# A mixing layer and two feed-forward layers on one core: features laid on the rows, with no turning on TensorE

## The chip, the cores and the metric

The kernel runs on one core of a Trainium2 chip. The metric is the device time in microseconds (us) of one execution. The kernel before takes 1403.92 us, the median of three runs (1402.54 to 1404.48). The profiled execution, from which all rows here come, took 1403.23 us, and its span from the first to the last instruction is 1401.4 us.

## The reference, cut to what matters

8192 tokens (2 sequences of 4096) of 192 features, in float32. First a causal mixing over 7 taps: 8 heads of 24 features each share a softmax weight for each tap. Then two feed-forward layers, 192 to 2048 to 192, with different functions between the two products.

```
w   = softmax(weight_gen over k)                  # [tokens, 8 heads, 7 taps]
mix[s, h, g] = sum_k w[s, h, k] * x_pad[s + k, h, g]   # 6 zero rows ahead of each sequence
h   = mix @ w_in1                                 # [8192, 2048]
g   = (a0 + a1 h + a2 h^2 + a3 h^3) / (1 + |b0| |h| + |b1| h^2 + 1e-6)
x2  = g @ w_out1
h   = x2 @ w_in2
y   = (h * clip(h + 3, 0, 6) / 6) @ w_out2
```

## The kernel before

**Precision by splitting.** TensorE is fed float32 values split into a rounded part ("hi") and the rest ("lo"). A product into a hidden layer is five matmuls of 128x128 by 128x512 (`first_product`, L502 to L506): hi by hi, hi by lo, lo by hi, and two for the features beyond 128 ("tail"). A product out of a hidden layer is five more (`second_product`, L510 to L514), into the two banks `acc_a` and `acc_b`. The tail rows carry the 64 features beyond 128 twice, so that one matmul does the work of two.

**Tiles and stages.** The tokens are cut into 16 blocks of 512. A block's hidden layer of 2048 is cut into 16 chunks of 128. Time is cut into segments `s` of 16 steps `c`. In segment `s` layer 1 works on block `s + 1` and layer 2 on block `s`, six chunks behind (`SHIFT`). Each full step so issues 20 matmuls: 5 into and 5 out of layer 1, 5 into and 5 out of layer 2. In segment -1 there is only layer 1 of block 0, and beside it the weights of layer 2 are loaded and split, and the mixing weights of all later tokens are normalised. Segments 1 to 12 are a hardware loop of two segments a turn, so 6 turns and 5 jumps back, on every engine; the others are unrolled.

**What a step does on the engines.** ScalarE (ACT): `den_num_start` reads the hidden chunk out of PSUM twice (L671, L672), `den_absolute` (L677), `den_log` (L682) and `recip_estimate` (L688) make a reciprocal as exp(-ln Q), `g1_round` (L695) and `g2_round` (L703) round the hidden activations, `gate_start` (L710) is layer 2's relu. VectorE (DVE): `den_sign` L843, `horner_v` L851, `horner_w` L858, `recip_t` L866, `recip_m` L874, `quotient` L885, and layer 2's `gate_h` L894. GpSimd (POOL): the two rests `g_lo`, L446 and L455. Each engine works strictly in the order in which its instructions are written out in `for c in range(NC)`; every hand-over is a semaphore.

**What a block adds.** Tokens are laid out with 4 tokens of each block on each of the 128 partitions, features along the row. POOL mixes in that layout: 7 products (L397) and 6 sums (L406, L411, L412), the weight of a head read again for each of its 24 features. TensorE then turns the mixed tile (`turn_mixed`, L615, 8 transposes), ACT and DVE round and subtract (L746, L916). The layer-1 sums are copied by ACT (L723, L726), the second bank is folded by a matmul with the matrix `fold` (`fold_layer1`, L577), and split (L731, L908). The result of layer 2 is copied (L716, L717), turned back (`turn_result`, L593 and L594, in steps 10 and 11), copied again (L740) and stored. All turned tiles pass through one PSUM bank, `turn`.

**PSUM.** There are eight banks: two each for `acc1` and `acc2`, two for `h1`, one for `h2`, one for `turn`. A layer-1 chunk occupies its `h1` bank from its first matmul until `quotient` has read it: TensorE's `layer1_in` waits for the quotient of two chunks before.

**Queues.** All DMAs are issued by SyncE (SP) on one queue in program order: per block one load of `x_win` and one store.

Of the kernel before, what the change touches and what calls it, by code (L numbers as in the profile page):

```python
# [7 lines left out]
F32 = mybir.dt.float32  # L26
# [4 lines left out]
TPB = 4  # L31
BLOCK = P * TPB
SHIFT = 6
Q_ONE = 1.0 + 1e-6


def build_program(nc, x, weight_gen, w_in1, w_out1, a, b, w_in2, w_out2, y):
    B, S, D = x.shape
    H, K = weight_gen.shape[2], weight_gen.shape[3]
    G = D // H  # L40
    F = w_in1.shape[1]
    TOKENS = B * S
    TPP = TOKENS // P
    NB = TPP // TPB
    NC = F // P
    D1 = P
    D2 = D - P
    HALO = K - 1
    NW = NC // 2
    CHUNKS = NB * NC  # L50
    assert D2 * 2 == P and TPP % TPB == 0 and NC == 16

    x_rows = x.rearrange("b s d -> (b s) d")
    x_own = x_rows.rearrange("(p t) d -> p t d", t=TPP)
    y_own = y.rearrange("(p t) d -> p t d", t=TPP)
    gen_own = weight_gen.rearrange("b s h k -> (b s) (h k)").rearrange("(p t) c -> p t c", t=TPP)

    with ExitStack() as ctx:
# [16 lines left out]

        x_win = sb("x_win", [P, HALO + TPB, D])
        mix_w = sb("mix_w", [P, TPP, H * K])
        mix_part = sb("mix_part", [P, TPB * D])
        mix_sum = sb("mix_sum", [P, TPB * D])
        mixed = sb("mixed", [P, TPB, 2 * P])  # L80
# [15 lines left out]
        late = sb("late", [P, 4 * BLOCK + TPB * D])  # L96
        gate = [late[:, i * BLOCK:(i + 1) * BLOCK] for i in (0, 1)]
        fin_a = late[:, 2 * BLOCK:3 * BLOCK]
        fin_b = late[:, 3 * BLOCK:4 * BLOCK]
        sum_b = fin_b  # L100
        y_out = late[:, 4 * BLOCK:]
        mix_part2 = y_out
# [6 lines left out]


        REST_PARTS = 4
        rest_tokens = (TPP - 2 * TPB) // REST_PARTS
        rest_n = rest_tokens * H
        rest_stats = y_out

        def rest_rows(part):
            start = 2 * TPB + part * rest_tokens
            return mix_w[:, start:start + rest_tokens, :]

        def rest_w(part):  # L120
            return rest_rows(part).rearrange("p t (h k) -> p (t h) k", k=K)

        def rest_stat(part):
            return rest_stats[:, part * rest_n:(part + 1) * rest_n]

        def rest_wide(part):
            return rest_stat(part).unsqueeze(2).to_broadcast([P, rest_n, K])

        ident = sb("ident", [P, P])
        fold = sb("fold", [P, P])  # L130
# [4 lines left out]
        h1 = [bank("h1_0"), bank("h1_1")]  # L135
        h2 = bank("h2")
        turn = bank("turn")
# [3 lines left out]
        gen_loaded = sem("gen_loaded")  # L141
        gen_rest_loaded = sem("gen_rest_loaded")
        x_first = sem("x_first")
        x_loaded = sem("x_loaded")
        staged0 = sem("staged0")
# [7 lines left out]
        x1_turned = sem("x1_turned")  # L153
        x2_folded = sem("x2_folded")
        y_turned = sem("y_turned")
# [7 lines left out]
        gate_ready = sem("gate_ready")  # L163
# [3 lines left out]
        g1_hi_ready = sem("g1_hi_ready")  # L167
        g2_hi_ready = sem("g2_hi_ready")
        x1_hi_ready = sem("x1_hi_ready")
        x2_hi_ready = sem("x2_hi_ready")  # L170
        sum_b_ready = sem("sum_b_ready")
        fin_ready = sem("fin_ready")
        y_ready = sem("y_ready")
# [6 lines left out]
        rest_recip = sem("rest_recip")  # L180
        den_signed = sem("den_signed")
# [6 lines left out]
        x1_lo_ready = sem("x1_lo_ready")  # L188
        x2_lo_ready = sem("x2_lo_ready")
        mix_added = sem("mix_added")  # L190

        const_step = sem("const_step")
        x_pad = sem("x_pad")
        rest_subtracted = sem("rest_subtracted")
        rest_scaled = sem("rest_scaled")
        mix_part_ready = sem("mix_part_ready")
        g1_lo_ready = sem("g1_lo_ready")
        g2_lo_ready = sem("g2_lo_ready")
        lo_split_pool = sem("lo_split_pool")

        def count(pair, per, block, more):
            return pair * (2 * per) + (block * per + more)


        FIRST, LOOP_FROM, PAIRS = -2, 1, (NB - 4) // 2
        LAST = NB

        def segments(eng, segment):  # L210
            for s in range(FIRST, LOOP_FROM):
                segment(0, s)
            with eng.Fori(0, PAIRS) as pair:
                segment(pair, LOOP_FROM)
                segment(pair, LOOP_FROM + 1)
            for s in range(LOOP_FROM + 2 * PAIRS, LAST + 1):
                segment(0, s)


# [7 lines left out]
        def is_block(n):  # L227
# [3 lines left out]
        PRODUCT1_LAG = 4  # L231
        PRODUCT2_LAG = 3
        RECIP_T_LAG = 1
        RECIP_M_LAG = 1
        QUOTIENT_LAG = 1
        G1_HI_LAG = 2
        G1_LO_LAG = 3
        GATE_LAG = 1
        G2_HI_LAG = 1
        G2_LO_LAG = 2  # L240


        SUMS1_COPY = 3
        SUMS1_REST = 3
        FOLD = 4
        FOLD_HI = 4
        FOLD_LO = 4
        SUMS2_COPY = 8
        Y_TURN = 10
        Y_COPY = 10  # L250
        Y_GAP = 1
        X_TURN = 12
        X_HI = 11
        X_LO = 12
        X_GAP = 1
        MIX_STEPS = 2 * K - 2
        MIX_ADDS = K
        HI_SPLITS = 4

        LO_OUT1, LO_IN2, LO_OUT2A, LO_OUT2 = 2, 6, 9, 12  # L260


        ROUND_STEPS = {0: ((0, 0), (0, 1)), 7: ((1, 0), (1, 1)), 10: ((2, 0),), 11: ((2, 1),), 14: ((3, 0), (3, 1))}
        EXP_STEPS = {0: (0,), 2: (1,), 4: (2,), 5: (3,)}

        LO_STEPS = {1: ((0, 0),), 2: ((0, 1),), 5: ((0, 2), (0, 3)), 11: ((2, 0),),
                    12: ((2, 1), (2, 2)), 14: ((3, 0), (3, 1)), 15: ((3, 2),)}
        SUB_STEPS = {1: (0,), 2: (1,), 3: (2, 3)}
        SCALE_STEPS = {10: (0,), 12: (1, 2), 14: (3,)}

        SUM_STEPS = {1: (0,), 3: (1,), 5: (2,), 6: (3,)}
        RECIP_STEPS = {7: (0,), 9: (1,), 10: (2, 3)}
        TAIL_STEPS = {8: (0, 1, 2, 3)}

        def gate_bank(s, c):

            last = s == NB or (s == NB - 1 and c >= SHIFT)
            return h1[c % 2] if last else h2
# [4 lines left out]

        @block.sync
        def _(sp):
            sp.dma_start(coef[:, 0:4], a.partition_broadcast(P)).then_inc(coef_loaded, 16)
            sp.dma_start(coef[:, 4:6], b.partition_broadcast(P)).then_inc(coef_loaded, 16)
            first = 2 * TPB
            sp.dma_start(mix_w[:, 0:first, :], gen_own[:, 0:first, :]).then_inc(gen_loaded, 16)


            def load_first(blk):
                old = HALO - TPB * blk
                if blk > 0:

                    sp.wait_ge(mix_part_ready, K * blk)
                before = x_own[:, TPP - old:TPP, :]
                for start in range(0, P, P // B):
                    n = P // B - 1
                    sp.dma_start(x_win[start + 1:start + 1 + n, 0:old, :],  # L300
                                 before[start:start + n, :, :]).then_inc(x_first, 16)
                sp.dma_start(x_win[:, old:HALO + TPB, :],
                             x_own[:, 0:HALO + TPB - old, :]).then_inc(x_first, 16)

            load_first(0)
            sp.dma_start(slot0, w_in1[0:P, :]).then_inc(staged0, 16)
            sp.dma_start(slot1[0:D2, :], w_in1[P:D, :]).then_inc(staged1, 16)
            sp.dma_start(slot1[D2:P, :], w_in1[P:D, :]).then_inc(staged1, 16)
            sp.dma_start(mix_w[:, first:, :], gen_own[:, first:, :]).then_inc(gen_rest_loaded, 16)
# [11 lines left out]
            load_first(1)  # L321
            sp.wait_ge(lo_split_pool, LO_OUT1)
            sp.dma_start(slot0, w_in2[0:P, :]).then_inc(staged0, 16)
            sp.wait_ge(lo_split_pool, LO_IN2)
            sp.dma_start(slot0[0:D2, :], w_in2[P:D, :]).then_inc(staged0, 16)
            sp.dma_start(slot0[D2:P, :], w_in2[P:D, :]).then_inc(staged0, 16)
            sp.wait_ge(tail_split, 4)
            sp.dma_start(w_slot(slot0), w_half(w_out2, 0)).then_inc(staged0, 16)
            sp.wait_ge(lo_split_pool, LO_OUT2A)
            sp.dma_start(w_slot(slot0), w_half(w_out2, 1)).then_inc(staged0, 16)  # L330

            def segment(pair, s):
# [656 lines left out]
```

## Time and profile before

| | |
|---|---|
| device time, median of 3 | 1403.92 us |
| profiled execution / its span | 1403.23 / 1401.4 us |
| busy: TensorE | 1285.1 us (92%) |
| busy: VectorE | 1245.5 us (89%) |
| busy: ScalarE | 1218.8 us (87%) |
| busy: GpSimd | 1030.8 us (74%) |
| moved by DMA | 32.09 MB, 23 GB/s over the span |
| mean granted TensorE clock | 0.985 |

Matmuls are pipelined: one is shown as some 0.39 us long, and the next begins 0.23 us after its start, so the distances between starts are what tells TensorE's pace. Three engines are close to full, so shares of busy time don't say which of them sets the pace; the waits and the distances between rows do.

### The profile page before, as it was taken

What the parts mean: (1) busy time and instruction counts of PE and PEld (TensorE: products, weight loads), DVE (VectorE), ACT (ScalarE), POOL (GpSimd) and SP (SyncE); (2) the same over time, 40 slices, a digit from 0 to 9 for tenths busy, and PEclk for the clock granted to TensorE, in tenths of its full rate; (3) what the DMA queues carried; (4) which work ended last, traced back from release to release, by engine and by line L of the source; (5) the groups of instructions that cost most, each with busy time, mean ns of one, the idle gap of its engine ahead of it and who ended that gap; (6) DMA issues with size and microseconds to landing.
All of it is one profiled execution on the core that took longest, in us unless ns stands there. A gap on an engine that the chain in (4) does not pass through costs nothing.

```text
span 1401.4 us, 19858 instructions
## 1 busy us (share of the span) xinstructions
PE 1285.1 (92%) x5472; PEld 994.5 (71%) x5472; DVE 1245.5 (89%) x1890; ACT 1218.8 (87%) x2211; POOL 1030.8 (74%) x761
## 2 busy tenths in 40 slices
PE   0556799999999999999999999999999999999998
PEld 0334477777777777777777777777777777777776
DVE  5897899999899998999899999999899999999932
ACT  2667899999899998999899998999899999999954
POOL 5658678788687868878687877868787887855554
PEclk9978999999999999999999999999999999999999
DMA  8121000100001010000101010010101000000000
GB/s 207 36 53 51 1 29 1 40 1 13 29 0 40 0 40 1 23 17 0 41 0 40 0 40 1 0 40 0 40 1 39 0 17 23 1 12 1 12 0 23
DMA packets 10334, 32.09 MB, mean 23 GB/s; under 512 B 1028, under 2 KB 5378, under 8 KB 9600
## 3 DMA queue, kind: packets, MB, share of 16 engines
q1 hardware_dynamic: 10240, 31.19, 7.0%
q14 instruction: 78, 0.64, 0.1%
q8 instruction: 16, 0.26, 0.1%
HBM read 24.89 MB, written 6.29 MB: 22 GB/s over the span
## 4 chain that ended last, share of the span: by engine, by line
PE 58%; DVE 17%; ACT 10%; issue 5%; DVEq 0%; POOL 0%; POOLq 0%; ACTq 0%
PE h L502 7%; PE acc_a L510 6%; PE acc_b L514 6%; PE acc_a L511 6%; PE acc_a L512 6%; PE acc_b L513 6%; PE h L504 5%; PE h L505 5%; PE h L503 5%; PE h L506 5%; DVE h L874 4%; DVE early L885 3%; DVE q_recip L866 3%; DVE early L843 3%; ACT g_hi L695 2%
## 5 line engine op out<-in xcount | busy, mean ns | idle before, releaser
L455 POOL TENSOR_TENSOR g_lo<-late,g_hi 128x512 fp32r<-128x512 f32 x256 | 332.1, 1297 | 300.8 <-ACT g_hi L703 300.5
L446 POOL TENSOR_TENSOR g_lo<-early,g_hi 128x512 fp32r<-128x512 f32 x256 | 333.2, 1302 | 32.3 <-ACT g_hi L695 32.3
L502 PE MATMUL h<-x_hi,w_in_hi 128*128 128x512 f32 x512 | 226.0, 441 | 71.6 <-DVE early L885 64.8
L894 DVE SCALAR_TENSOR_TENSOR late<-late,h 128x512 f32<-128x512 f32 x256 | 175.6, 686 | 97.7 <-ACT late L710 79.6
L510 PE MATMUL acc_a<-g_hi,w_out 128*128 128x512 f32 x512 | 213.0, 416 | 2.0 <-ACT late L717 1.1
L502 PEld LDWEIGHTS h<-x_hi,w_in_hi 128*128 128x128 f32 x512 | 97.0, 190 | 155.1 <-DVE early L885 130.7
L695 ACT CAST g_hi<-early 128x512 fp32r<-128x512 f32 x256 | 159.9, 625 | 50.9 <-PE acc_b L514 49.1
L505 PE MATMUL h<-x_tail_hi,w_in_tail 128*128 128x512 f32 x512 | 203.8, 398 | 0.0
L504 PE MATMUL h<-x_hi,w_in_lo 128*128 128x512 f32 x512 | 203.6, 398 | 0.0
L503 PE MATMUL h<-x_lo,w_in_hi 128*128 128x512 f32 x512 | 203.4, 397 | 0.0
L506 PE MATMUL h<-x_tail_lo,w_in_tail 128*128 128x512 f32 x512 | 203.1, 397 | 0.0
L511 PE MATMUL acc_a<-g_hi,w_out 128*128 128x512 f32 x512 | 202.9, 396 | 0.0
L512 PE MATMUL acc_a<-g_lo,w_out 128*128 128x512 f32 x512 | 202.2, 395 | 0.0
L513 PE MATMUL acc_b<-g_hi,w_out 128*128 128x512 f32 x512 | 201.6, 394 | 0.0
L514 PE MATMUL acc_b<-g_lo,w_out 128*128 128x512 f32 x512 | 201.3, 393 | 0.0
L858 DVE SCALAR_TENSOR_TENSOR early<-early,coef,h 128x512 f32<-128x512 f32 x256 | 191.3, 747 | 8.6
L843 DVE SCALAR_TENSOR_TENSOR early<-early,coef,h 128x512 f32<-128x512 f32 x256 | 189.8, 741 | 3.2 <-ACT early L672 3.1
L874 DVE SCALAR_TENSOR_TENSOR h<-early,coef,h 128x512 f32<-128x512 f32 x256 | 191.9, 750 | 0.0
L866 DVE SCALAR_TENSOR_TENSOR q_recip<-early,h 128x512 f32<-128x512 f32 x256 | 174.9, 683 | 14.6 <-ACT h L688 10.0
L688 ACT ACTIVATE h<-early 128x512 f32<-128x512 f32 x256 | 154.2, 602 | 25.4 <-DVE early L858 23.9
L672 ACT ACTIVATE early<-h,coef 128x512 f32<-128x512 f32 x256 | 175.5, 686 | 0.0
L885 DVE SCALAR_TENSOR_TENSOR early<-q_recip,h 128x512 f32<-128x512 f32 x256 | 174.1, 680 | 1.6 <-POOL g_lo L446 1.5
(83 smaller groups left out, 2536.1 us busy)
## 6 DMA issues: line engine op xcount, KB each, us to landing
x_win<-in_x SPq DMA_DIRECT2D x14, 960.0 KB, 4.9
out_y<-late SPq DMA_DIRECT2D x16, 384.0 KB, 2.6
late<-in_moe_w_out SPq DMA_DIRECT2D x3, 768.0 KB, 4.7
late<-in_moe_w_in SPq DMA_DIRECT2D x2, 1024.0 KB, 9.2
mix_w<-in_weight_gen SPq DMA_DIRECT2D x1, 1568.0 KB, 21.3
early<-in_moe_w_in SPq DMA_DIRECT2D x2, 512.0 KB, 16.8
late<-in_moe_w_in SPq DMA_DIRECT2D x2, 512.0 KB, 6.0
early<-in_moe_w_out SPq DMA_DIRECT2D x1, 768.0 KB, 4.8
```

The lines of the kernel that those rows point to most:

```text
L446: nc.gpsimd.tensor_tensor(g1_lo[p][:, :], neg_g[p], g1_hi[p][:, :].bitcast(F32), ALU.subtract).then_inc(g1_lo_ready, 1)
L455: nc.gpsimd.tensor_tensor(g2_lo[p][:, :], gate[p], g2_hi[p][:, :].bitcast(F32), ALU.subtract).then_inc(g2_lo_ready, 1)
L502: pe.matmul(out[:, :], w_hi[:, cols], hi[:, :], start=True, stop=False)
L503: pe.matmul(out[:, :], w_hi[:, cols], lo[:, :], start=False, stop=False)
L504: pe.matmul(out[:, :], w_lo[:, cols], hi[:, :], start=False, stop=False)
L505: pe.matmul(out[:, :], w_tail[:, cols], tail_hi[:, :], start=False, stop=False)
L506: return pe.matmul(out[:, :], w_tail[:, cols], tail_lo[:, :], start=False, stop=True)
L510: pe.matmul(acc[0][:, :], w[:, c, 0:P], hi[:, :], start=first, stop=False)
L511: pe.matmul(acc[0][:, :], w[:, c, 2 * P:2 * D], hi[:, :], start=False, stop=False)
L512: pe.matmul(acc[0][:, :], w[:, c, 0:P], lo[:, :], start=False, stop=last)
L513: pe.matmul(acc[1][:, :], w[:, c, P:2 * P], hi[:, :], start=first, stop=False)
L514: return pe.matmul(acc[1][:, :], w[:, c, P:2 * P], lo[:, :], start=False, stop=last)
```

## The change

Host code now hands the kernel `x` with features on the rows and tokens along them, already cut into windows (256 tokens and the 6 before them), and `weight_gen` with (head, part of the tokens) on the rows. The output is written with features on rows, and turned by the host.

- **Mixing.** A block's 192 features by 512 tokens lie as 128 rows by 512 and, for the last 64 features, 128 rows by 256 (two halves of the tokens). One product per tap covers all 768 columns, now with a full tile of weights. The normalised weights go to a DRAM tensor `mix_weights` and come back by broadcasting DMAs that copy a head's row over its 24 features: 12 DMAs for taps 0 to 3 and 12 for taps 4 to 6 in each block. Block 0 is mixed by DVE, all others by POOL.
- **No turning.** `turn_mixed`, `fold_layer1`, `turn_result` and the matrices `ident` and `fold` are gone. The mixed tail is brought to both halves of the rows by eight small DMAs per block (`copy_tail`). The fold of the second bank is done by two ACT copies that move 64 rows to the other 64 (`sum_part`) and one DVE addition (`x2_tail`); the fold of the result likewise (`y_part`, `y_tail`).
- **A third h1 bank** takes the place of `turn`; `layer1_in` waits for the quotient of three chunks before.
- **New orders** on all engines, other lags, and the hardware loop has 6 segments a turn and 2 turns (SP is unrolled).

```diff
-        h1 = [bank("h1_0"), bank("h1_1")]
+        h1 = [bank("h1_0"), bank("h1_1"), bank("h1_2")]
         h2 = bank("h2")
-        turn = bank("turn")
...
+    LOOP_FROM, LOOP_BLOCKS, LOOPS = 1, 6, 2
...
+        PRODUCT_STEPS = {0: (0, 1), 2: (2,), 3: (3,), 5: (4,), 7: (5,), 9: (6,)}
+        ADD_STEPS = {1: (1,), 3: (2,), 4: (3,), 6: (4,), 8: (5,), 11: (6,)}
...
+            def load_mix_w(turn, blk, taps, loaded):
+                for head, row, rows, token, tokens, col in MIX_ROWS:
+                    src = mix_weights[head, taps, bass.ds(count(turn, BLOCK, blk, token), tokens)]
+                    sp.dma_start(mix_w[row:row + rows, taps, col:col + tokens],
+                                 src.partition_broadcast(rows)).then_inc(loaded, 16)
...
+            sp.wait_ge(soft_step, 6)
+            store_weights(first_w, 0, FIRST_N, first_stored)
+            sp.wait_ge(first_stored, 16 * H)
+            load_mix_w(0, 0, slice(0, A_TAPS), mix_w_a)
+            load_mix_w(0, 0, slice(A_TAPS, K), mix_w_b)
...
+            def copy_tail(turn, blk):
+                hi, lo = x1[blk % 2][2], x1[blk % 2][3]
+                sp.wait_ge(x1_tail_hi_ready, count(turn, 1, blk, 1))
+                for rows in (0, D2):
+                    for half in (0, 1):
+                        sp.dma_start(hi[rows:rows + D2, half * HALF:(half + 1) * HALF].bitcast(F32),
+                                     tail_hi[half * D2:(half + 1) * D2, :].bitcast(F32)).then_inc(tail_hi_copied, 16)
...
+                nc.gpsimd.tensor_tensor(
+                    out[:, :].rearrange("p (g n) -> p g n", n=HALF),
+                    x_win[:, :].rearrange("p (g n) -> p g n", n=WIN)[:, :, k:k + HALF],
+                    mix_w[:, k, :].rearrange("p (g n) -> p g n", n=HALF), ALU.mult).then_inc(mix_product_ready, 1)
...
-                        if has1(s, c, 2):
-                            pe.wait_ge(g1_ready, count(pair, NC, s + 1, c - 1))
+                        if has1(s, c, 3):
+                            pe.wait_ge(g1_ready, count(turn, NC, s + 1, c - 2))
...
                 for c in range(NC):
-
                     layer1_in(c)
-                    fold_layer1(c)
-                    turn_mixed(c)
-                    layer2_out(c)
-                    layer1_out(c)
-                    turn_result(c)
                     layer2_in(c)
+                    layer1_out(c)
+                    layer2_out(c)
...
+                        act.activation(sum_part[0:D2, :], acc1[1][D2:P, :], ACT.Copy,
+                                       scale=-1.0).then_inc(sum_part_ready, 1)
+                        act.activation(sum_part[D2:P, :], acc1[1][0:D2, :], ACT.Copy,
+                                       scale=-1.0).then_inc(sum_part_ready, 1)
...
+                for c in range(NC):
+                    den_start(c)
+                    den_log(c)
+                    gate_start(c)
+                    recip_estimate(c)
+                    num_start(c)
+                    copy_layer1(c)
+                    round_x2_tail(c)
+                    round_mixed(c)
+                    g1_round(c)
+                    g2_round(c)
+                    copy_result(c)
+                    den_absolute(c)
+                    prepare(c)
...
+                for c in range(NC):
+                    den_sign(c)
+                    rest_layer1(c)
+                    horner_v(c)
+                    add_result(c)
+                    recip_m(c)
+                    horner_w(c)
+                    quotient(c)
+                    gate_h(c)
+                    recip_t(c)
+                    prepare(c)
```

The last two lists are ScalarE's and VectorE's. In the new order `den_log` and `recip_estimate` handle the chunk of the step before, `recip_m` and `quotient` too, and `layer2_in` comes one step later than it did. `rest_layer1` (step 3) makes both the lo part of the first 128 features and `x2_tail`, and TensorE's next `layer1_out` with p = 0 (step 4) waits for it.

## Rows read from the trace of the kernel before

**Rows 1.** View by windows (busy us and count per engine, TensorE clock, DMA), by stage.

```profile
20.00:40.00 20.00, 2.23 (x8) 1.43 (x8) 15.88 (x9) 5.62 (x5) 12.53 (x7) 1.00 0.78 248
...
43.80:133.90 90.10, 53.34 (x149) 36.60 (x149) 79.45 (x112) 65.47 (x108) 62.87 (x45) 0.84 0.14 40
133.90:211.40 77.50, 65.60 (x259) 48.41 (x258) 71.45 (x110) 67.07 (x120) 55.42 (x41) 0.94 0.04 13
534.40:613.80 79.40, 76.98 (x335) 59.97 (x336) 75.22 (x117) 74.54 (x137) 61.85 (x46) 1.00 0.05 18
1254.70:1332.00 77.30, 76.50 (x333) 59.97 (x332) 73.07 (x114) 72.44 (x135) 40.31 (x32) 1.00 0.02 6
1332.00:1394.80 62.80, 60.76 (x266) 47.90 (x264) 19.60 (x29) 32.92 (x56) 32.76 (x26) 1.00 0.02 7
```

**Rows 2.** View of the waits: who waited for whom, us, times, longest.

```profile
POOL g_lo L455 <- ACT g_hi L703: 300.5, 239, 3.5
PEld h L502 <- DVE early L885: 130.7, 194, 7.1
DVE late L894 <- issue: 11.6, 5, 2.5
```

**Rows 3.** Timeline (start, length in us, engine, line): TensorE in a steady step.

```profile
702.65 0.49 PE L502 MATMUL h<-x_hi,w_in_hi 128*128 128x512 f32 x1
...
703.90 0.39 PE L510 MATMUL acc_a<-g_hi,w_out 128*128 128x512 f32 x1
...
707.10 0.39 PE L506 MATMUL h<-x_tail_lo,w_in_tail 128*128 128x512 f32 x1
...
707.33 0.49 PE L502 MATMUL h<-x_hi,w_in_hi 128*128 128x512 f32 x1
```

**Rows 4.** Timeline: two starts on ACT, then four on DVE, same step.

```profile
704.54 0.58 ACT L671 ACTIVATE early<-h 128x512 f32<-128x512 f32 x1
...
705.02 0.69 ACT L672 ACTIVATE early<-h,coef 128x512 f32<-128x512 f32 x1
...
704.67 0.68 DVE L866 SCALAR_TENSOR_TENSOR q_recip<-early,h 128x512 f32<-128x512 f32 x1
...
705.26 0.75 DVE L874 SCALAR_TENSOR_TENSOR h<-early,coef,h 128x512 f32<-128x512 f32 x1
...
707.18 0.68 DVE L851 TENSOR_TENSOR early<-early,h 128x512 f32<-128x512 f32 x1
...
707.89 0.75 DVE L858 SCALAR_TENSOR_TENSOR early<-early,coef,h 128x512 f32<-128x512 f32 x1
```

**Rows 5.** Timeline: TensorE after layer 1 has ended, two chunks.

```profile
1370.54 0.39 PE L502 MATMUL h<-x_hi,w_in_hi 128*128 128x512 f32 x1
...
1372.80 0.39 PE L502 MATMUL h<-x_hi,w_in_hi 128*128 128x512 f32 x1
```

**Rows 6.** View by line and form (busy us, mean ns | idle before): the transposes.

```profile
L615 PE MATMUL turn<-ident,mixed 128*128 128x128 f32 x128 | 20.6, 286 | 37.5 <-DVE mixed L821 36.0 <-DVE x_lo L916 1.5
```

**Rows 7.** View by line and form: GpSimd's rests, products and sums.

```profile
L446 POOL TENSOR_TENSOR g_lo<-early,g_hi 128x512 fp32r<-128x512 f32 x256 | 333.2, 1302 | 32.3 <-ACT g_hi L695 32.3
L397 POOL TENSOR_TENSOR mix_part<-x_win,mix_w 128x768 f32<-128x768 f32 x93 | 144.5, 1554 | 1.8 <-DVE mix_sum L816 1.8
L406 POOL TENSOR_TENSOR mix_sum<-mix_sum,mix_part 128x768 f32<-128x768 f32 x75 | 139.6, 1861 | 0.0
```

**Rows 8.** Timeline: the start of the kernel, SP's queue and DVE.

```profile
1.66 0.42 SPq L289 DMA_DIRECT2D mix_w<-in_weight_gen  x1
...
6.78 0.62 DVE L791 TENSOR_REDUCE early<-mix_w 128x64 f32<-128x448 f32 x1 [6.78 <-DMA mix_w<-in_weight_gen]
...
14.51 2.21 DVE L816 TENSOR_TENSOR mix_sum<-mix_sum,mix_part 128x768 f32<-128x768 f32 x1 [3.64 <-POOL mix_part L397]
...
20.99 0.95 DVE L816 TENSOR_TENSOR mix_sum<-mix_sum,late 128x768 f32<-128x768 f32 x1
```

**Rows 9.** View of the DMAs: out<-in, issuer, count, KB each, us to landing.

```profile
out_y<-late SPq DMA_DIRECT2D x16, 384.0 KB, 2.6
```

More of the change, by code:

```diff
@@ L212, in segments @@
                 segment(0, s)
[L213 to L216, printed above, removed]
+            with eng.Fori(0, LOOPS) as turn:
+                for s in range(LOOP_FROM, LOOP_FROM + LOOP_BLOCKS):
+                    segment(turn, s)
+            for s in range(LOOP_FROM + LOOP_BLOCKS * LOOPS, LAST + 1):
                 segment(0, s)
@@ L280, in build_program, with add_steps @@
+        def add_steps(s):
+            return {3: (1,), 5: (2,), 6: (3,), 7: (4,), 9: (5,), 10: (6,)} if s == -1 else ADD_STEPS
         block_ctx = nc.Block()
         block = ctx.enter_context(block_ctx)
+        MIX_ROWS = []
+        for head in range(H):
+            lo_row, hi_row = head * G, (head + 1) * G
+            if lo_row < P:
+                MIX_ROWS.append((head, lo_row, min(hi_row, P) - lo_row, 0, BLOCK, 0))
+            if hi_row > P:
+                row = max(lo_row, P)
+                for half in (0, 1):
+                    MIX_ROWS.append((head, half * D2 + row - P, hi_row - row, half * HALF, HALF, BLOCK))
@@ L350, in _ @@
+            for s in range(FIRST, LAST + 1):
+                segment(0, s)
+            sp.wait_ge(y_stored, 32 * NB)
         @block.gpsimd
         def _(pool):
[L353 to L360 removed]
@@ L598, in turn_mixed @@
[L598 to L617 removed]
+                if s == FIRST:
+                    return
@@ L742, in round_mixed @@
-                def round_mixed(c):
-                    if c in (X_HI, X_HI + X_GAP) and is_block(s + 2):
-                        part = (c - X_HI) // X_GAP
-                        act.wait_ge(x1_turned, count(pair, 2, s + 2, part + 1))
-                        act.copy(x1[s % 2][2 * part][:, :], turn[:, :]).then_inc(x1_hi_ready, 1)
+                            for part in (2, 3):
+                                act.wait_ge(rest_stored[part], 16 * H)
+                        else:
+                            act.wait_ge(x2_tail_ready, count(turn, 1, s - 1, 1))
@@ new lines, in rest_layer1, with add_result @@
+                        if s > 0:
+                            dve.wait_ge(x2_tail_lo_ready, count(turn, 1, s - 1, 1))
+                        dve.scalar_tensor_tensor(x2_tail, acc1[1][:, :], -1.0, sum_part, ALU.mult,
+                                                 ALU.add).then_inc(x2_tail_ready, 1)
+                def add_result(c):
+                    if c == SUMS2 and is_block(s - 1):
+                        dve.wait_ge(y_part_ready, count(turn, 1, s - 1, 1))
+                        if is_block(s - 2):
+                            dve.wait_ge(y_stored, count(turn, 32, s - 2, 32))
+                        dve.scalar_tensor_tensor(y_tail, acc2[1][0:D2, :], 1.0 / 6.0, y_part, ALU.mult,
+                                                 ALU.add).then_inc(y_tail_ready, 1)
```

920 lines of the change are left out of this document (468 added, 452 removed).

## The prediction

> **What bounds the kernel now.** I read the windows by stage first. The first hidden chunk reaches ScalarE at 43.8 us, block 0 (layer 1 only) holds the kernel until 133.9, block 1 until 211.4; a block in the middle takes 79.4 (534.4 to 613.8), the last block's 16 steps 77.3, the drain of layer 2 62.8, and from 1394.8 the last result is turned and stored in 6.6 [rows 1]. The reader is to see that TensorE is busy 76.98 of 79.4 while VectorE has 75.22 and ScalarE 74.54: three engines nearly full, so the share alone names none.
>
> The waits come next: TensorE's weight loads for the hidden product stand 130.7 us behind the quotient L885, in 194 places [rows 2]; that is the h1 bank coming free. The timeline of one step shows the price. From one layer-1 L502 to the next it takes 4.68 us. Between 703.90 and 707.10 there are 14 distances of 0.2286, so 20 matmuls without a hole are 4.57; the hole is 0.11 [rows 3]. In the drain, with one layer left, ten matmuls take 2.26, or 4.53 for twenty [rows 5]: 4.5 to 4.6 is TensorE's floor, and nothing in the change alters it. 16 steps of 4.68 are 74.9; the remaining 4.5 of the 79.4 lie at the steps with folds and turns: transposes of 0.286 [rows 6], and waits for ACT and DVE to empty the one bank `turn` between halves. Last, five jumps back of the loop leave DVE without instructions for 11.6 us, 2.3 each [rows 2].
>
> **The change part by part, middle blocks.** Turns and folds leave TensorE: up to 4.5 per block. The third bank gives the quotient a whole step more: the hole of 0.11 goes, 1.8 per block. That leaves 16 x 4.57 = 73.1. What is late next? DVE: an instruction of 0.68 gives the engine over after 0.59 [rows 4], 0.09 before its recorded end, so one of 0.75 takes 0.66. Four of 0.59 and three of 0.66 are 4.34 a step; the stall of L858 on L851 directly before it (0.71 between starts, rows 4) goes, since `recip_m` now stands between. 16 x 4.34 and three block instructions (x2 lo, `x2_tail`, `y_tail`, 0.6 each) make 71.3. ACT: 137 instructions in the block hold it for 74.54, 0.54 each [rows 1]; without dependent neighbours 0.48 to 0.57 (0.48 behind the first of rows 4), and 136 remain (128 and eight of the block): 65 at 0.48, 74 at 0.54; I take 71, as most are behind independent ones now. So both fit under 73.1, by some 2 us each. GpSimd: 32 rests of 1.30 are 41.7. A product has no repeated operand any more, so I price it as the sum of two full tiles, 1.86 instead of 1.55 [rows 7]: 7 x 1.86 + 6 x 1.86 = 24.2, and three splits of 1.30, 1.30 and 0.7, 3.3: 69 (67 with products at 1.55). GpSimd waits 300.5 us for L703 today [rows 2], about 19 a block, which the 7 more can use. Steps 0 and 3 hold two mixing instructions and step 6 a mixing one and a split, so it falls behind by up to 3.5; `g1_lo` is needed one step and a half later than it can be made, so this stays hidden; if it did not, it would cost those 3.5.
>
> A new wait is `layer1_out` with p = 0 behind `x2_tail`. After the last sum of step 3, ACT makes x2 hi and the two half copies (3 x 0.48), the second ends 0.6 after its start, DVE adds in 0.69: 1.44 + 0.1 + 0.69 = 2.3 and hand-overs, while TensorE still has `layer2_out` of step 3 and both input products of step 4, 15 matmuls or 3.4. It fits by about a microsecond less ACT's own lateness; queued behind it are `layer2_out` and all of TensorE. ACT falls 1.4 behind in step 3, DVE as much, against a slack of 2 steps less the chain (about 1.5) at h1. I add 0.8 per block for what doesn't fit: 73.9 (bounds 73.1 and 77.5; the upper one is DVE and ACT never catching up).
>
> DMA: per block SP issues 35 instead of 2 transfers, at 0.42 [rows 8] 15 us of a block, and moves 2.75 MB of weights more: at the 248 GB/s of 20 to 40 us [rows 1] 11 us. Taps 0 to 3 of the next block may be loaded from step 4 on and are needed 12 steps later, taps 4 to 6 after step 14 and needed in step 5: 7 steps, 32 us, for 12 issues of 0.42, 5 us of transfer and a landing of 2.6 [rows 9]. Hidden; each of these could be three times dearer.
>
> The Trainium skill ("DMA: Bandwidth & Descriptors", Why a DMA increments its semaphore by 16) states that a DMA is spread over the largest number up to 16 that divides the outer dimension of both sides: the 24 rows of a head use 12 engines. By it the loads run at three quarters of the rate, 15 instead of 11 us a block, still hidden, and the start is 2 us later.
>
> Loop: one jump back instead of five, 4 x 2.3 = 9.2 saved; were the jump out of a longer body dearer, it would be one.
>
> **The start.** Softmax begins at 6.78 and its load is now first (issued at 0.75 rather than 1.66 [rows 8]): it ends at 10.0. New on the path: 8 stores (3.4 issued, 2.6 landing): 16.3; 12 loads with 1.57 MB, 6.6 and 2.6: 25.5; 12 more by 30.5. Then DVE mixes alone, 13 instructions, each behind the one before: 0.95 while GpSimd stands, 2.21 beside a product of GpSimd [rows 8]. GpSimd has nothing to do there, so 13 x 0.98 = 12.7: ends at 38.5. Rounding, rest, eight copies and landing: 0.4 + 0.7 + 3.4 + 2.6 = 45; TensorE's first five, at 0.43 each as in block 0, 48.3 instead of 43.8: +4.5 (bounds 0 and +16, with transfers at half the rate or DVE at 2.2).
>
> **Block 0** took 90.1, of it DVE 79.45 [rows 1]. DVE has the same preparation and a block less dependent: some 76; the third bank loosens the chain, and new waits on loads for block 1 stand in GpSimd's queue ahead of its rests. I take 87 (bounds 77 and 100).
>
> **Sum**, in us of the span: 43.8 + 4.5 = 48.3; block 0 87; block 1 75 (77.5 now; its first steps have only layer 1); 13 blocks of 73.9, 960.7, and one jump 2.3; the last block's 16 steps 73.6 (77.3); the drain 60.5 (62.8, less turns and fold); the end 4.8 (6.6: two copies, an addition and a store of 2.6 without turning). Together 1312.2; the profiled execution is 1.8 longer than its span, 1314.0, and 0.7 under the median, within what I can tell: 1314.
>
> **Rivals.** (a) The h1 wait is a symptom: DVE and ACT set 4.68 and only the turns go. For it: their 75.22 and 74.54. Against: the holes on TensorE, the stall of L858, and DVE's idle 0.2 a step. Then a block is 74.9 and the time 15 x 1.0 more: 1329. (b) The new wait on `x2_tail`, or ACT's crowded steps 3 and 8, stop TensorE each block by 2 to 3 us: 76.4, 15 x 2.5 more, 1352. For it: ACT is nearly full, three copies stand in a row. (c) Slower than before: GpSimd becomes the bound, in the products that read shifted windows and a full second tile. Its block is 56.1 (41.7, 11.2, 3.3) + 7p; it passes today's 79.4 at p = 3.33, and at p = 4 a block is 84.1 and the time 15 x 10.2 more, 1467. Against: 768 columns with two full operands take 1.86 now. (d) Better: nothing is lost at steps 3 and 8 and block 0 comes down to 78: 1314 - 12 - 9 = 1293. (e) The change doesn't do what it says, mixing weights arriving late: needs the DMAs three times dearer; in (c)'s class by size.
>
> The Trainium skill ("SBUF — State Buffer", Who interferes with whom) states that a DVE instruction with two SBUF inputs and a GpSimd instruction that reads SBUF lock each other out. The trace agrees: 0.95 against 2.21 for the same sum [rows 8]. It speaks for DVE mixing block 0 while GpSimd stands still; with both at work the start would be 16 us later.
>
> **How the numbers follow.** Forecast 0.52 (own range 1302 to 1325), (a) 0.20, (b) 0.13, (c) and (e) 0.04, (d) 0.11. The range holds the forecast, (a), (d) and the milder half of (b): 1292 to 1346. 0.2% is about what a measurement can tell from no change. Faster 0.96, the same 0.01, slower 0.03.
>
> **What would show it.** In the changed profile: a middle step of 4.57 with L502's successor no longer behind the quotient; a block of 73 to 75 without a transposing step; POOL products of 1.8 to 1.9; one "issue" gap; first chunk near 48 us. Wrong it is if a middle block is over 76, if TensorE waits for `x2_tail`, if GpSimd is busy over 95%, or if block 0 lasts over 100.

## The result, and the profile after

The changed kernel takes 1347.5 us (median of four runs, 1343.8 to 1349.6) against 1404.2 (the kernel before, now four runs): ratio 0.9593 [0.9569, 0.9617], 4.1% faster. Forecast were 1314 us, 6.4%. The direction is right, and the time lies 1.5 us above the range. The profiled execution, the fastest of the four, took 1343.76; its span is 1341.9, where the sum had 1312.2: 29.7 us are to be found.

The windows of the kernel after (busy us and count per engine, granted clock, DMA share, GB/s), cut where the first hidden chunk reaches ScalarE in each block, as in [rows 1]:

```profile
54.10:154.60 100.50, 50.95 (x140) 33.92 (x139) 82.17 (x111) 62.61 (x107) 68.77 (x46) 0.69 0.53 113
154.60:224.80 70.20, 60.48 (x242) 45.64 (x243) 67.49 (x106) 65.08 (x121) 59.72 (x43) 0.98 0.28 59
826.00:900.70 74.70, 74.70 (x321) 60.01 (x321) 72.71 (x116) 72.97 (x137) 66.37 (x49) 1.00 0.26 56
1199.40:1274.00 74.60, 74.60 (x322) 59.92 (x321) 72.64 (x116) 72.42 (x135) 42.12 (x34) 1.00 0.02 6
1274.00:1341.90 67.90, 61.02 (x256) 47.14 (x254) 22.23 (x33) 34.86 (x59) 34.87 (x28) 0.98 0.04 12
```

The reader is to see in the third row that TensorE is busy for 74.70 of 74.70 us: nothing makes it wait any more. All the same the block is 0.8 longer than forecast. The timeline of one steady step says why:

```profile
834.00 0.40 PE L544 MATMUL h<-x_hi,w_in_hi 128*128 128x512 f32 x1
834.24 0.39 PE L545 MATMUL h<-x_lo,w_in_hi 128*128 128x512 f32 x1
834.47 0.39 PE L546 MATMUL h<-x_hi,w_in_lo 128*128 128x512 f32 x1
...
836.34 0.39 PE L552 MATMUL acc_a<-g_hi,w_out 128*128 128x512 f32 x1
...
838.67 0.39 PE L544 MATMUL h<-x_hi,w_in_hi 128*128 128x512 f32 x1
```

Twenty matmuls take 838.67 - 834.00 = 4.67 without a hole, 0.2333 each. Before they stood 0.2286 apart in the step of [rows 3] and 0.2267 in the drain [rows 5]. The hole of 0.11 is gone, and nearly all of it has come back as slower matmuls at the same full clock. Here is the sum, term by term, in us of the span:

| term | forecast | measured | difference |
|---|---|---|---|
| start, to the first chunk on ACT | 48.3 | 54.1 | +5.8 |
| block 0 | 87 | 100.5 | +13.5 |
| block 1 | 75 | 70.2 | -4.8 |
| 13 blocks and one jump back | 963.0 | 974.6 | +11.6 |
| last block's 16 steps | 73.6 | 74.6 | +1.0 |
| drain and end | 65.3 | 67.9 | +2.6 |

The start, from the timeline (SPq rows: the DMA queue issuing, with its count):

```profile
15.25 11.05 SPq L292 DMA_DIRECT2D mix_w<-mix_weights  x24
...
29.80 0.96 DVE L839 TENSOR_TENSOR mix_sum<-x_win,mix_w 128x768 f32<-128x768 f32 x1 [12.92 <-DMA mix_w<-mix_weights]
...
38.48 0.96 DVE L839 TENSOR_TENSOR mix_part<-x_win,mix_w 128x768 f32<-128x768 f32 x1 [1.89 <-DMA mix_w<-mix_weights]
...
44.87 2.42 SPq L345 DMA_DIRECT2D x_tail_hi<-tail_hi  x4
```

Softmax ended at 10.2 (forecast 10.0) and the loads are issued from 15.25, on time. But mixing starts at 29.80 instead of 25.5 and waits 1.89 more for the second half. The windows show that the DMA engines are at work, and slow:

```profile
20.00:25.00 5.00, 0.00 (x0) 0.00 (x0) 0.00 (x0) 0.00 (x0) 0.00 (x0) 1.00 0.80 139
25.00:30.00 5.00, 0.00 (x0) 0.00 (x0) 0.20 (x1) 0.00 (x0) 0.00 (x0) 1.00 0.96 155
```

I had priced the loads at the 248 GB/s of [rows 1]; they ran at 139 here (from 26.35 on, loads of the weights of layer 2 run beside them). A rule had been weighed here too: by the Trainium skill ("DMA: Bandwidth & Descriptors", Why a DMA increments its semaphore by 16) 24 rows use twelve engines. The trace agrees. Every DMA here leaves a few small packets: the six copies of 64 rows that run between 44.8 and 49.8 us leave 96, sixteen each. Between 15 and 44.8 us there are the 24 broadcasting loads and four other DMAs, 28 in all:

```profile
DMA packets 4456, 5.13 MB, mean 172 GB/s; under 512 B 360, under 2 KB 3304, under 8 KB 4456
```

At sixteen each, 448 packets would be small. With twelve for each of the eighteen loads of 24 rows, eight for each of the two of 8 rows and sixteen for the other eight DMAs it is 360, as in the row. The share of 0.80 says nothing against it: loads of 16 rows run beside the others from 20 us on, and the share is a sum over packets that can overlap (it is 1.05 in e12 from 22 to 30 us). Between 16 and 20 us, when nearly all under way are of 24 rows, it is 0.53:

```profile
16.00:20.00 4.00, 0.00 (x0) 0.00 (x0) 0.88 (x1) 0.00 (x0) 0.00 (x0) 1.00 0.53 148
```

By the prediction's own figure the rule is worth 2 of the 5.8 us; the rest is the rate at which these loads ran even so, and what sets it stays open.

Block 0 is the dearest miss. Its waits (who waited for whom, us in all, times, longest):

```profile
PEld acc_a L552 <- POOL g_lo L472: 36.5, 10, 8.6
ACT early L693 <- DVE early L863: 25.6, 11, 8.8
PE h L544 <- DVE early L900: 19.0, 6, 6.2
POOL late L503 <- DVE late L933: 16.2, 3, 9.6
POOL mix_sum L423 <- issue: 9.2, 1, 9.2
```

TensorE stands behind GpSimd's rests L472; GpSimd in turn stands behind VectorE's maximum L933, which is preparation of the later blocks' mixing weights and comes ahead of the rests in GpSimd's queue, and 9.2 under "issue", at the instruction that waits for the loads for block 1 (`mix_w_a`). A row of the worst step, then, and the form of the two reductions by line (busy us, mean ns; L933 is the maximum, L942 the sum), which read their taps strided now:

```profile
125.47 1.85 POOL L503 TENSOR_TENSOR late<-late 128x784 f32<-128x784 f32 x1 [9.56 <-DVE late L933]
```

```profile
L933 DVE TENSOR_REDUCE late<-late 128x112 f32<-128x784 f32 x4 | 6.0, 1516 | 0.0
L942 DVE TENSOR_REDUCE late<-late 128x112 f32<-128x784 f32 x4 | 6.1, 1522 | 0.0
```

The same reductions took 960 ns before, over contiguous taps: eight of 0.56 more are 4.5, and six of the eight lie in block 0 (3.4).

### The profile page after: what moved, and what is told of

Same layout as the page of the kernel before. It is cut to its first block, busy times and chain, and to the rows that moved or that the text cites. A ratio compares the mean times of both kernels' runs of the same rounds, so it can differ in the third digit from the quotient of the medians.

```text
span 1341.9 us, 20224 instructions
## 1 busy us (share of the span) xinstructions
PE 1221.3 (91%) x5120; PEld 968.3 (72%) x5120; DVE 1215.4 (91%) x1883; ACT 1192.0 (89%) x2195; POOL 1072.0 (80%) x779
## 3 DMA queue, kind: packets, MB, share of 16 engines
q1 hardware_dynamic: 60272, 75.16, 25.5%
## 4 chain that ended last, share of the span: by engine, by line
PE 84%; DVE 5%; issue 3%; ACT 2%; POOL 2%; DMA 2%; SPq 1%; POOLq 0%; ACTq 0%; DVEq 0%
PE acc_a L552 9%; PE h L544 9%; PE acc_a L554 8%; PE acc_b L556 8%; PE acc_b L555 8%; PE acc_a L553 8%; PE h L548 8%; PE h L545 8%; PE h L547 8%; PE h L546 8%; DMA mix_w<-mix_weights 1%; DVE q_recip L884 1%; SPq L292 1%; DVE early L869 1%; DVE early L863 1%
## 5 line engine op out<-in xcount | busy, mean ns | idle before, releaser
L472 POOL TENSOR_TENSOR g_lo<-early,g_hi 128x512 fp32r<-128x512 f32 x256 | 334.2, 1306 | 140.0 <-ACT g_hi L714 139.9
L544 PE MATMUL h<-x_hi,w_in_hi 128*128 128x512 f32 x512 | 207.6, 406 | 79.0 <-DMA x_tail_lo<-tail_lo 51.5
L552 PE MATMUL acc_a<-g_hi,w_out 128*128 128x512 f32 x512 | 206.0, 402 | 37.3 <-POOL g_lo L472 33.3
L553 PE MATMUL acc_a<-g_hi,w_out 128*128 128x512 f32 x512 | 203.8, 398 | 0.0
L693 ACT ACTIVATE early<-early 128x512 f32<-128x512 f32 x256 | 162.3, 634 | 32.9 <-DVE early L863 29.6
L733 ACT CAST g_hi<-late 128x512 fp32r<-128x512 f32 x256 | 161.3, 630 | 33.2 <-PE acc_b L556 19.0
```

The lines of the kernel that those rows point to most:

```text
L472: nc.gpsimd.tensor_tensor(g1_lo[p][:, :], neg_g[p], g1_hi[p][:, :].bitcast(F32), ALU.subtract).then_inc(g1_lo_ready, 1)
L544: pe.matmul(out[:, :], w_hi[:, cols], hi[:, :], start=True, stop=False)
L552: pe.matmul(acc[0][:, :], w[:, c, 0:P], hi[:, :], start=first, stop=False)
L553: pe.matmul(acc[0][:, :], w[:, c, 2 * P:2 * D], hi[:, :], start=False, stop=False)
```

## Experiments

**First: is it the chip, or where the tiles lie?** The changed kernel's `x_win` is 3144 bytes a partition, no multiple of 64, and with the tiles next to it it has moved every streamed tile behind it against the weight tiles, which lie ahead. Four kernels on one chip: the changed one again, the one before again, the changed one with 56 bytes of filling, and the one before with 32.

```diff
 e1_aligned (from the changed kernel)
-        x_win = sb("x_win", [P, 3 * WIN])
+        x_win_all = sb("x_win", [P, 3 * WIN + 14])
+        x_win = x_win_all[:, 0:3 * WIN]
 e2_before_shifted (from the kernel before)
+        shift = sb("shift", [P, 8])
         x_win = ...
```

> Only x_win is 14 numbers longer per row, so that all tiles behind it (x1, x2, g_hi, g_lo) begin on a multiple of 64 bytes instead of 32 beyond one. Theory P (place): a moving tile that begins 32 bytes off costs TensorE one more fetch per matmul, 0.2333 us from start to start instead of 0.2267. Then the distance falls to 0.2267 to 0.229, a middle block from 74.67 to about 73, and the time by 15 blocks x 1.7 plus the drain, 25 to 32 us, to about 1318. Theory S (saturation): TensorE without holes runs at 0.2333 whatever the tiles, because it never rests. Then the distance stays 0.2333 and the time within 0.2% of the changed kernel. Theory D (DMA traffic, 57 against 23 GB/s): the same as S.

> The kernel before with 32 more bytes ahead of x_win, so that the tiles behind it begin 32 bytes beyond a multiple of 64. Theory P: distances between matmuls become 0.2333, also in the drain, where ten now take 2.26; twenty and the hole of 0.11 are 4.7 to 4.78 instead of 4.66, and the time rises by 10 to 34 us. Theories S and D: nothing moves, 1404 within 0.2%.

> The changed kernel as it is, on the same chip as the other three. If the slower distance were a matter of the chip that took its profile, it would be 0.227 to 0.229 here. Theories P, S and D: 0.2333 again and 1344 to 1350.

> The kernel before as it is, for its profile on this chip. Theories P, S and D: distances of 0.2267 to 0.2286 and 1402 to 1406. If the chip were the cause: 0.2333.

Measured: e3 1348.1 with 0.2333 between matmuls, e4 1407.3 (one run) with the distances of the kernel before, on one chip; so it isn't the chip. e2, which differs from the kernel before by 32 empty bytes a partition alone, takes 1412.4 (ratio 1.0059 [1.0043, 1.0076]), 8 us more where 10 to 34 were expected. From its timeline, to be laid beside [rows 3]:

```profile
837.97 0.39 PE L512 MATMUL acc_a<-g_hi,w_out 128*128 128x512 f32 x1
...
841.23 0.39 PE L503 MATMUL h<-x_hi,w_in_hi 128*128 128x512 f32 x1
```

These are 14 distances without a hole, 3.26 or 0.2329 each, where the kernel before had 0.2286. So the place counts. But e1 gives 1341.7 instead of the 1318 hoped for, only 6.5 us less than e3, and its twenty matmuls still take 4.67:

```profile
835.86 0.40 PE L545 MATMUL h<-x_hi,w_in_hi 128*128 128x512 f32 x1
...
840.53 0.40 PE L545 MATMUL h<-x_hi,w_in_hi 128*128 128x512 f32 x1
```

A multiple of 64 bytes is not the point, or not all of it.

**Second: the old places exactly; another multiple; and what bounds a block apart from TensorE.**

```diff
 e5_placed (from the changed kernel)
-        x_win = sb("x_win", [P, 3 * WIN])
+        x_win_all = sb("x_win", [P, 3 * WIN + 110])
+        x_win = x_win_all[:, 0:3 * WIN]
 ...
-        tail_lo = sb("tail_lo", [P, HALF], F32R)
 ...
+        tail_lo = sb("tail_lo", [P, HALF], F32R)
         coef = ...
 e6_before_640 (from the kernel before)
+        shift = sb("shift", [P, 160])
 e7_light (from e1)
-  pe.matmul(out[:, :], w_tail[:, cols], x_tail_hi[:, :], start=False, stop=False)
-  return pe.matmul(out[:, :], w_tail[:, cols], x_tail_lo[:, :], start=False, stop=True)
+  return pe.matmul(out[:, :], w_tail[:, cols], x_tail_hi[:, :], start=False, stop=True)
 e8_two_banks (from e1)
-            return h1[((s + 1) * NC + c) % 3]
+            return h1[((s + 1) * NC + c) % 2]
 ...
-                            pe.wait_ge(g1_ready, count(turn, NC, s + 1, c - 2))
+                            pe.wait_ge(g1_ready, count(turn, NC, s + 1, c - 1))
```

> The changed kernel with x_win padded and tail_lo moved, so that every tile that TensorE streams (x1, x2, g_hi, g_lo) has the address of the kernel before, or one 4096 bytes on. Theory P2 (the place counts beyond its remainder by 64): the distance between matmuls falls from 0.2325 to 0.2267 to 0.229, a middle block from 74.5 to about 73, the time to about 1318. Theory S (a TensorE that never rests runs at 0.2333 for another reason than place): 0.2323 to 0.2333 as in e1_aligned, and 1338 to 1344.

> The kernel before with its tiles moved by 640 bytes, to where e1_aligned has them: a multiple of 64 all the same. P2: distances of 0.2323 to 0.2333 instead of 0.2267 to 0.229, and 1409 to 1415. S: 0.2267 to 0.229 and 1402 to 1407.

> e1_aligned without the last matmul of each input product (tail weights by the low part of the tail), in both layers: 18 matmuls a step, so TensorE has holes. S: with rests between, the distance inside a group falls to 0.2267 to 0.229. P2: it stays 0.2323 or more. Beside it the block time tells what VectorE and ScalarE alone allow: 71 to 72 by my counts; if (a) of the rivals had been right, 74 or more.

> e1_aligned with layer 1 on two h1 banks again: layer1_in waits for the quotient of two chunks before. My theory of the change: the third bank lets TensorE run without holes, so with two there are holes at L545 behind L901 and a middle block is 76 to 80. Rival: the new orders alone do it, and the block stays 74.5.

e5 takes 1318.9 (1317.5 to 1319.9; ratio 0.938 [0.936, 0.9401]), some 29 us less than the same code in the places the change gave it. Its window of a middle block and its steady timeline:

```profile
813.40:886.30 72.90, 72.90 (x322) 59.95 (x321) 72.39 (x117) 72.01 (x138) 66.26 (x49) 1.00 0.26 59
```

```profile
836.06 0.39 PE L545 MATMUL h<-x_hi,w_in_hi 128*128 128x512 f32 x1
...
840.62 0.39 PE L545 MATMUL h<-x_hi,w_in_hi 128*128 128x512 f32 x1
```

Twenty matmuls take 4.56, and 19 distances from 839.48 on take 4.31, 0.2268 each. Just behind a hole they are longer even here: in e5 the eight from 835.12 to 836.98 take 1.86, 0.2325 each. The kernel before does the same:

```profile
702.98 0.39 PE L503 MATMUL h<-x_lo,w_in_hi 128*128 128x512 f32 x1
...
705.06 0.39 PE L510 MATMUL acc_a<-g_hi,w_out 128*128 128x512 f32 x1
```

Nine distances up to 705.06 take 2.08 (0.2311), the nine from there to 707.10 [rows 3] take 2.04 (0.2267). So the 0.2286 of [rows 3] is a mean of two stretches, and twenty matmuls without any hole, in these places, are 4.53 as in the drain [rows 5]. In the other places (the changed kernel, e1, e6) the distance doesn't fall with the way from the last hole.

e6 puts 640 bytes ahead in the kernel before, a multiple of 128. Its one run took 1409.0, 3 above the median of the seven runs beside it and 0.6 above the slowest, so the time says little; the distances do, with 18 of them in 4.18 (0.2322). So no round number alone makes it fast, either.

e7 leaves out the product of the tail's remainder (each chunk has four input matmuls instead of five): 1303.2. TensorE has room now (70.66 busy of 72.30), and the distance stays at 0.232 to 0.233: it is not the fullness of the engine that slows it, and theory S is out. And the block is 72.3:

```profile
804.20:876.50 72.30, 70.66 (x289) 52.81 (x289) 72.15 (x117) 71.41 (x137) 66.20 (x49) 1.00 0.26 59
```

VectorE is busy 72.15 of it: that is what DVE and ACT allow, 1 us over my 71.3 and 0.6 under e5's block. e8 goes back to two banks for layer 1 and takes 2342 us (ratio 1.667). A stretch of it, somewhat more than one block (136 to 140 each):

```profile
826.00:975.00 149.00, 98.47 (x334) 73.76 (x335) 76.24 (x120) 78.72 (x143) 66.53 (x49) 0.87 0.14 33
```

```profile
DVE late L909 <- ACT late L725: 71.1, 17, 4.9
POOL g_lo L473 <- ACT g_hi L715: 66.4, 14, 7.8
PEld h L545 <- DVE early L901: 59.4, 17, 4.9
ACT early L682 <- PE h L549: 56.9, 17, 4.2
```

Three of the four waits come 17 times in as many steps, and a step takes 8.6. The new engine orders put the quotient of a chunk behind the first work on the next one, and with two banks the chunk after that can't enter TensorE before this quotient, so the engines take turns. The third bank isn't an addition to the new orders but their condition. I had expected 76 to 80 for a block.

**Third: what about the place; and block 0, the jump and the start.** All from e5.

```diff
 e9_shift_all: 128 bytes ahead of the first weight tile; all tiles move together
+        shift = sb("shift", [P, 32])
 e10_prep: the preparation's due steps
-        TAIL_STEPS = {8: (0, 1, 2, 3)}
-        MAX_STEPS = {8: 2, 10: 3}
-        SUB_STEPS = {9: 2, 11: 3}
+        TAIL_STEPS = {8: (0, 1), 9: (2, 3)}
+        MAX_STEPS = {6: 2, 7: 3}
+        SUB_STEPS = {9: 2, 10: 3}
 ...
 e11_one_turn
-LOOP_FROM, LOOP_BLOCKS, LOOPS = 1, 6, 2
+LOOP_FROM, LOOP_BLOCKS, LOOPS = 1, 12, 1
 e12_plain: block 0's weights from rows of x, in two plain loads
-            load_mix_w(0, 0, slice(0, A_TAPS), mix_w_a)
-            load_mix_w(0, 0, slice(A_TAPS, K), mix_w_b)
+            sp.dma_start(mix_w[:, 0:A_TAPS, :]..., x[:, 0:A_TAPS * MIX]).then_inc(mix_w_a, 16)
+            sp.dma_start(mix_w[:, A_TAPS:K, :]..., x[:, A_TAPS * MIX:K * MIX]).then_inc(mix_w_b, 16)
```

> e5_placed with 128 bytes ahead of the first weight tile, so that weights and streamed tiles all move by 128 together. In e5 both begin at 128 beyond a multiple of 256, in the slower e1 the streamed tiles at 0 and the weights at 128. Theory R (what counts is the place of the streamed tile relative to the weights): distances stay 0.2267 and the time 1319. Theory A (the absolute place): 0.2325 and about 1341.

> e5_placed with another order of the preparation in segment -1: VectorE takes the maxima of parts 2 and 3 two and three steps earlier, GpSimd subtracts the last a step earlier, the tail split is spread over two steps. Theory Q (block 0 is long because GpSimd's in-order queue stands behind VectorE's maxima, 16 us, with the rests for TensorE behind it): block 0 falls from 100 by 6 to 13 us and the time with it. Rival: VectorE's own load (82 of 100) sets it, and block 0 falls by less than 3.

> e5_placed with segments 1 to 12 in one turn of the loop instead of two of six: no jump back. The jump shows as 4.6 us in block 7 and 2.9 in block 8. Theory: both go, 7 us, about 1312. Rival: the gap is the fetch of new instructions, which straight code needs too, and less than 2 us go.

> e5_placed with block 0's mixing weights (24 broadcasting loads, 12 of 16 engines for a head of 24 rows) read by two plain loads of 128 rows and the same bytes from x: block 0 is mixed with wrong weights. Theory: the broadcasting loads' rate (2.75 MB in 23 us, 118 GB/s) makes the start late; with plain ones taps 0 to 3 are there at 24 instead of 29.8, and the first chunk comes at 46 to 48 instead of 54. Rival: the loads share the DMA engines with later ones and the rate is the HBM's: less than 3 us.

e9 takes 1318.7 in its one run, with ten distances in 2.27:

```profile
843.54 0.39 PE L546 MATMUL h<-x_hi,w_in_hi 128*128 128x512 f32 x1
...
845.81 0.39 PE L554 MATMUL acc_a<-g_hi,w_out 128*128 128x512 f32 x1
```

Moving everything by 128 bytes changes nothing, so it isn't the absolute place. All kernels, by where a streamed tile and the weights lie, in bytes by 256:

| kernel | streamed | weights | apart | us between matmuls |
|---|---|---|---|---|
| before, e5 | 128 | 128 | 0 | 0.2267 to 0.2286 |
| e9 | 0 | 0 | 0 | 0.2267 |
| e1 | 0 | 128 | 128 | 0.2323 to 0.2335 |
| e6 | 0 | 128 | 128 | 0.2323 |
| e2 | 160 | 128 | 32 | 0.2329 to 0.2333 |
| after, e3 | 224 | 128 | 96 | 0.2333 |

Fast are the rows where the two are alike, slow the four where they are not. Since 128 apart is slow, the period is over 128 bytes; that it is 256, and not a larger power that the fast rows also share, isn't settled; nor is the mechanism. Each of these edits moves all tiles behind `x_win` together. That the streamed ones are what counts is an inference: of the tiles behind `x_win`, TensorE reads no others in the changed kernel.

e10: 1321.2 and block 0 100.7, nothing gained. The wait that I aimed at fell from 16.2 in the changed kernel to 3.2, and another came in its place, GpSimd for ScalarE's rounding of `w_out`, in the waits of block 0:

```profile
PEld h L545 <- DVE early L901: 28.1, 7, 6.1
PEld acc_a L553 <- POOL g_lo L473: 26.5, 7, 10.8
POOL w_out L445 <- ACT w_out L652: 22.7, 2, 19.1
```

e11: 1313.3. The blocks at the jump, 77.43 and 75.71 in e5, are 72.74 and 72.85, so the one jump cost 7.4 there. Its one run is 5.6 under e5's median, as block 0 was 1.8 longer (kernels with the same block 0 have 100.0 to 101.8 for it, so this is spread from run to run). e12: 1310.1. Mixing starts at 21.94 and the first chunk comes at 44.4 instead of 53.9, and block 0 stays at 100.5: the 24 small loads cost 9.5, and block 0 doesn't hang on the start. e12 changes the number of loads, the rows of each and the length of a piece (12 KB instead of 1 to 2 KB) at once, so which of them is slow isn't told.

```profile
15.24 0.35 SPq L318 DMA_DIRECT2D mix_w<-in_x  x1
...
21.94 0.96 DVE L842 TENSOR_TENSOR mix_sum<-x_win,mix_w 128x768 f32<-128x768 f32 x1 [5.09 <-DMA mix_w<-in_x]
```

**Fourth: the best version, and block 0 with parts of its preparation left out.** e13 is e11 again, in five rounds; the others start from it.

```diff
 e14_no_max
-        MAX_STEPS = {8: 2, 10: 3}
-        SUB_STEPS = {9: 2, 11: 3}
+        MAX_STEPS = {}
+        SUB_STEPS = {}
 ...
 e15_raw: the same, and
-        EXP_STEPS = {0: 0, 1: 1, 9: 2, 12: 3}
-        SUM_STEPS = {1: 0, 2: 1, 10: 2, 13: 3}
-        SCALE_STEPS = {2: 0, 3: 1, 12: 2, 14: 3}
+        EXP_STEPS = {}
+        SUM_STEPS = {}
+        SCALE_STEPS = {}
 ...
```

> e5_placed with the loop in one turn (e11), timed in rounds: both gains together, 1312 to 1315, against 1319 with two turns.

> e13 without the maxima and their subtraction for the mixing weights of the later tokens (VectorE 4 x 1.5, GpSimd 4 x 1.8 to 2.3 us; in exact arithmetic the weights are the same). Theory Q2: block 0 is set by the in-order handing of the preparation between VectorE, ScalarE and GpSimd, so with one round trip per part less it falls by 8 to 14, to 1299 to 1305. Rival C (clock: TensorE at half its clock in most of block 0, granted 0.70, sets it): less than 3.

> e13 without any preparation of the later tokens' mixing weights (loaded and stored as they are; all blocks but the first two get unnormalised weights). What block 0 lasts without it: Q2 expects 75 to 82 of the 100, the rest being layer 1's own 61 on VectorE, the weight splits and the mixing of block 1; C expects 95 or more.

e13: 1314.2 (1312.3 to 1315.8; ratio 0.9347 [0.9327, 0.9367]), 4.7 us less than e5, though the two intervals still touch. e14: 1306.7 (0.9304 [0.9282, 0.9326]); block 0 is 95.0, 5.6 less (8 to 14 were expected), and the step of 13.13 us at step 9 is 8.65. e15: 1296.5, and block 0 takes 81.8, 19 less. Block 0 in e13, e14 and e15 (busy of TensorE, its weight loads, VectorE, ScalarE, GpSimd; clock, DMA):

```profile
55.10:155.80 100.70, 51.69 (x140) 34.88 (x139) 82.08 (x111) 62.43 (x107) 68.58 (x46) 0.69 0.52 111
53.90:148.90 95.00, 53.36 (x140) 36.47 (x138) 74.24 (x108) 62.57 (x107) 60.39 (x42) 0.68 0.56 120
54.50:136.20 81.70, 49.50 (x140) 34.33 (x138) 63.97 (x95) 59.51 (x102) 52.15 (x37) 0.75 0.62 142
```

VectorE has 7.8 and 18.1 us less to do than in e13, and the block is 5.6 and 18.9 shorter. So the rival written down for e10, that VectorE's own load sets the block, fits these two runs as well as the theory of hand-overs does: both edits take away work and hand-overs together. Against it as the only cause: e10 took 2.8 us off VectorE in the block (81.6 to 78.8) and gained nothing.

The clock is still at a mean of 0.75 in e15. In the changed kernel the clock is at its lower level, 1.2 GHz, for 24 us on end, and TensorE rests more than half of them:

```profile
59.00:82.90 23.90, 9.63 (x20) 6.12 (x20) 20.80 (x29) 14.75 (x26) 15.35 (x10) 0.50 0.84 169
```

So the lower clock goes with a starved TensorE here. That it sets the block is out: with it the removed preparation would have gained less than 3. What it adds to the block isn't measured.

## Why the prediction was right, and where it was wrong

**Right** were the direction and the reasons for the gain, though no run divides the gain between the missing turns, the third bank and the new orders; e8 shows only that the orders need the bank. Turns and folds are gone and no step is long by them; the hidden product no longer waits for the quotient in the middle blocks. Over the whole run its wait is

```profile
PEld h L544 <- DVE early L900: 35.1, 29, 6.6
```

where it was 130.7 in 194 places [rows 2], and most of what is left lies in block 0. Products on GpSimd take 1.71 to 1.75 in the mean (forecast 1.86, bounds 1.55 and 1.86), so it is busy 66.37 of 74.70; rival (c) is out. TensorE waits nowhere in a middle block, so rival (b), the wait on `x2_tail`, is out, and the 0.8 I added for it wasn't spent: in e5 the block is 72.86 against 73.9. The DMAs of a middle block, 56 GB/s at a share of 0.26, are hidden. Rival (a), DVE and ACT set the step, is out by e7: they allow 72.3.

**The step that failed** is "4.5 to 4.6 is TensorE's floor, and nothing in the change alters it". The change altered it, through a thing that I hadn't read in the diff as one at all: the size of `x_win` and the new tail tiles, and with them the place of every streamed tile. It costs up to 0.0066 a matmul (0.0057 in the mean of a block), 1.8 us a block and some 26 in all; e3 and e5 stand 29 apart. In the prediction's own terms the floor of 16 x 4.57 = 73.1 became 74.7, and the 0.8 a block that wasn't spent on `x2_tail` hid half of it. With the tiles in their old places the kernel is at 1318.9, inside the forecast's own 1302 to 1325. [Rows 3, 5] stood before me with 0.2286 and 0.2267, and I took two unequal distances of one instruction for one floor without asking what sets it. Part of the answer stood in the same step: the distance is longer behind a hole.

**Block 0** was mis-sized as much, 100.5 against 87 and just over the upper bound; "over 100" was one of the signs of being wrong. I took 76 for VectorE's work and it was 82.2, of which the strided reductions are 3.4; and I named the waits on loads in GpSimd's queue, but gave them nothing. e15 shows that preparing the later weights costs about 19 us of the block, e14 that the maximum and its subtraction are 5.6 of them. How this divides between hand-overs and VectorE's work isn't settled: e10 moved the hand-over and gained nothing.

**The start** was mis-sized by 5.8: the transfers, priced at 248 GB/s, ran at 118 (2.75 MB in 23 us) over the whole and at 139 to 155 in the windows shown. The bound of +16, which I kept for half the rate or a slower VectorE, holds. VectorE at 0.96 a mixing instruction while GpSimd rests was as forecast, and so was the reason ([rows 8]).

**The jump** cost 3.8 in the profiled run and 7.4 in e5, not 2.3 [rows 2]: with a body of six blocks rather than two it is dearer. I had written down that a longer body may make it dearer, and put it off as one jump only. **Block 1** was 4.8 shorter than I took it: its first steps have only layer 1, and I take it that this is unhindered now; no run tests it. **Drain and end** took 2.6 more; they are 66.8 in e5, so 1.1 of it is from the slower matmuls.

Together: the distance of the matmuls is 14 x 1.81 = 25.3 in the blocks (74.67 less e5's 72.86) and 1.1 in the drain, block 0 is 13.5, the start 5.8, the jump 1.5, the rest of the end 1.5; against them stand 4.8 at block 1 and 13 x 1.04 + 0.7 = 14.3 by which e5's blocks are shorter than the 73.9 and 73.6 I took. That is 29.6 of the 29.7.

## What to carry to other kernels

Where TensorE is the bound, read the distance between the starts of its matmuls before and after, and not only its waits: an edit that changes a tile's size moves all tiles behind it, and here 32 empty bytes made the kernel 0.6% slower. Put the streamed tiles at the same remainder as the weights (by 256 bytes held here) and measure once with them there. Price a load on the starting path by a landing of the same shape, count the first block with the preparation in each engine's queue in order, and don't take a loop's jump out of a longer body at the shorter one's price.

## What the runs showed of the hardware that was not expected

- Matmuls of 128x512 stand 0.2267 apart where streamed and weight tiles lie alike by 256 bytes, and 0.2323 to 0.2335 where they don't, 2.5 to 3%, at the full clock and with the engine full or with room (e7). Even in the fast places they stand some 0.2325 apart for about nine matmuls behind a hole (before, e5).
- Of 24 loads that spread one row each over 8 to 24 partitions, 2.75 MB in all, the first twelve had landed 14.5 us after the first was issued; one plain load of the same bytes, the first of two, was in use 6.7 us after its issue (e12).
- A reduction over a strided inner axis took 1.52 instead of 0.96 (128x784) on VectorE.
- With two banks instead of three for layer 1 the new orders took 1.67 times the time of the kernel before (e8).
